# Top-k attention and two MLPs on one core: copies to x, reciprocals and weight stores put later in their queues

## What is computed

```python
scores = q @ k.T / sqrt(64)                       # per head, 576 x 576
kth    = np.partition(scores, -32)[..., -32:-31]   # the 32nd largest of each row
scores = np.where(scores >= kth, scores, -1e9)
attn   = exp(scores - max); attn /= attn.sum(-1) + 1e-9
x      = (attn @ v), heads side by side            # 2304 x 512
gate   = sigmoid(x @ w_gate); val = x @ w_val      # w: 512 x 1536
x      = (gate * val) @ w_out                      # 1536 x 512
h      = x @ w_in                                  # 512 x 2048
out    = relu(h)**2 @ w_out2                       # 2048 x 512
```

## Time and profile before

| | |
|---|---|
| median of 3 runs | 1241.93 us |
| the profiled execution's own time | 1240.17 us |
| its span, first to last instruction | 1238.4 us |
| busy: TensorE / VectorE / ScalarE / GpSimd | 94% / 68% / 60% / 51% of the span |
| mean granted TensorE clock | 0.983 of full speed |

### The profile page before, as it was taken

How to read it: one execution, slowest core, us unless ns; L and a number is a source line. 1 busy time by engine, 2 the same in 40 slices (tenths; PEclk the granted TensorE clock), 3 DMA queues, 4 the chain that set the end, 5 groups by cost and what they waited for, 6 DMA issues and landing times.

```text
span 1238.4 us, 21824 instructions
## 1 busy us (share of the span) xinstructions
PE 1163.2 (94%) x7520; PEld 1004.4 (81%) x7520; DVE 841.3 (68%) x1756; ACT 741.5 (60%) x1758; POOL 628.2 (51%) x539
## 2 busy tenths in 40 slices
PE   3559999989989999999999999999999999999999
PEld 2337888978878999998987777777887888899998
DVE  7788898776678779899967867996565767001140
ACT  5677778766576677677665556765455466112130
POOL 4776678675476456366545434654254256112030
PEclk9969999999989999999999999999999999999999
DMA  9677777776666867665755455556454454577774
GB/s 358 246 259 228 266 258 238 273 270 239 229 245 224 303 201 240 203 218 186 232 192 182 164 190 170 190 184 212 151 199 154 164 170 159 182 241 255 251 256 145
DMA packets 90397, 270.13 MB, mean 218 GB/s; under 512 B 10032, under 2 KB 16176, under 8 KB 90288
## 3 DMA queue, kind: packets, MB, share of 16 engines
q1 hardware_dynamic: 90288, 268.74, 64.5%
HBM read 228.33 MB, written 40.37 MB: 217 GB/s over the span
## 4 chain that ended last, share of the span: by engine, by line
PE 78%; ACT 8%; POOL 5%; issue 3%; DMA 2%; DVE 1%; SPq 1%; ACTq 0%; POOLq 0%
PE ps L582 19%; PE ps L584 18%; PE ps L583 18%; PE ps L523 7%; PE ps L568 7%; PE ps L484 5%; PE ps L500 4%; POOL below L828 2%; DMA wring<-w_in 2%; ACT below L619 2%; ACT scores L614 1%; ACT below L626 1%; POOL ring L823 1%; ACT probs L633 1%; POOL full_buf L868 1%
## 5 line engine op out<-in xcount | busy, mean ns | idle before, releaser
L828 POOL TENSOR_TENSOR below<-scores,below 128x576 f32<-128x576 f32 x144 | 205.5, 1427 | 274.4 <-ACT below L626 273.6
L762 DVE MAX8 top<-work 128x8 f32<-128x576 f32 x432 | 312.2, 750 | 5.0
L582 PE MATMUL ps<-xy_hi,ring 128*128 128x512 f32 (+2 forms) x800 | 290.1, 363 | 4.4 <-ACT act_buf L692 2.4
L584 PE MATMUL ps<-xy_hi,ring 128*128 128x512 f32 (+2 forms) x800 | 282.1, 353 | 0.0
L583 PE MATMUL ps<-xy_lo,ring 128*128 128x512 f32 (+2 forms) x800 | 281.6, 352 | 0.0
L764 DVE MATCH_REPLACE8 work<-top,work 128x576 f32<-128x576 f32 x288 | 213.9, 743 | 0.0
L582 PE MATMUL ps<-g_hi,ring 128*128 128x384 f32 (+2 forms) x560 | 202.8, 362 | 2.7 <-POOL g_lo L857 2.7
L584 PE MATMUL ps<-g_hi,ring 128*128 128x384 f32 (+2 forms) x560 | 198.0, 354 | 0.0
L583 PE MATMUL ps<-g_lo,ring 128*128 128x384 f32 (+2 forms) x560 | 197.7, 353 | 0.0
L833 POOL TENSOR_TENSOR probs<-probs,rinv 128x576 f32<-128x576 f32 x128 | 154.9, 1210 | 62.8 <-DVE rinv L777 62.7
L582 PEld LDWEIGHTS ps<-xy_hi,ring 128*128 128x128 f32 x800 | 150.7, 188 | 24.1 <-issue 6.2
(11 more groups left out here) (58 smaller groups left out, 1723.9 us busy)
## 6 DMA issues: line engine op xcount, KB each, us to landing
ring<-w_split SPq DMA_DIRECT2D x318, 512.0 KB, 3.8
wring<-w_in SPq DMA_DIRECT2D x113, 256.0 KB, 4.2
w_split<-stage SPq DMA_DIRECT2D x46, 512.0 KB, 4.6
w_split<-ring SPq DMA_DIRECT2D x22, 512.0 KB, 3.0
vt<-v_in SPq DMA_DIRECT2D x16, 480.0 KB, 4.6
heads_in<-qk_in SPq DMA_DIRECT2D x16, 336.0 KB, 4.4
vt<-v_in SPq DMA_DIRECT2D x16, 320.0 KB, 3.4
heads_in<-qk_in SPq DMA_DIRECT2D x16, 304.0 KB, 4.2
```

The source lines that it names most:

```text
L582: nc.tensor.matmul(dst, w_hi, hi[:, k, 0:WIDTH[c]], start=first, stop=False)
L584: mm = nc.tensor.matmul(dst, w_lo, hi[:, k, 0:WIDTH[c]], start=False, stop=final)
L762: nc.vector.max(out=best, in_=sc if step == 0 else wk).then_inc(sel_step[t % 2], 1)
L828: nc.gpsimd.tensor_tensor(out=below[:, t % 2, :], in0=scores[:, t % PLACES, :], in1=below[:, t % 2, :], op=ALU.subtract).then_inc(mask_don ...
```

## The change

Three edits, none of which adds or takes away an operation.

- SyncE: the store of a block split on the way goes out at block k for job k + AHEAD - STORE_LAG = k + 2, where it was k + 5.
- ScalarE, slots before 15: `copy_x` of the unit whose product TensorE makes in slot s stood at the end of slot s; it now stands in slot s+1 behind `find_below` and `enlarge`. The last unit of chunk 0 (slot 14) stays.
- VectorE, slots from 15 on: `invert` (the reciprocal) stood behind the first two steps of the selection and ahead of the MLP's work left from the slot before; it now stands behind that work and behind the third step. Slots before 15 had that order already.

```diff
@@ mlp_dma (SyncE) @@
-                    if k + AHEAD in SPLIT_OF and JOBS[k + AHEAD][0] == NW:
-                        store_parts(k + AHEAD)
+                    done = k + AHEAD - STORE_LAG
+                    if done in SPLIT_OF and JOBS[done][0] == NW:
+                        store_parts(done)
@@ ScalarE, slots before MLP_AT[0] @@
                     enlarge(s - MASK)
+
+                if s - 1 in PROD_AT:
+                    copy_x(PROD_AT[s - 1])
                 if s - 1 in SCORE_AT:
                     for t in tiles_of(SCORE_AT[s - 1]):
                         copy_scores(t)
-                if s in PROD_AT and s == MLP_AT[0] - 1:
+                last = s == MLP_AT[0] - 1
+                if last:
                     copy_pt(PROD_AT[s])
                 if 0 <= s - MASK:
                     exp(s - MASK)
-                if s in PROD_AT and s < MLP_AT[0] - 1:
+                if s in PROD_AT and not last:
                     copy_pt(PROD_AT[s])
                 for k in SPLIT_AT.get(s, []):
                     split_weights(k)
-                if s in PROD_AT:
+                if last:
                     copy_x(PROD_AT[s])
@@ VectorE @@
                 select_both(s, [0, 1])
-                if s in NORM_AT and s >= MLP_AT[0]:
-                    invert(NORM_AT[s])
                 for c, n in blocks_of(SHARES[s - 1][2]) if s else []:
                     evac(c, n)
                 select_both(s, [2])
-                if s in NORM_AT and s < MLP_AT[0]:
+                if s in NORM_AT:
                     invert(NORM_AT[s])
```

## The result

| kernel | median us | runs | ratio to the kernel before, 95% interval |
|---|---|---|---|
| before | 1246.32 | 6 (1241.38 to 1248.59) | 1 |
| all three edits | 1237.78 | 6 (1237.31 to 1238.64) | 0.9939 [0.9916, 0.9962] |

The change is faster by 0.4 to 0.8%, 5 to 10 us. The forecast was 1216 us, a gain of 24, with a range of 1206 to 1230: too much, by a factor of three. The profiled execution of the kernel before took 1240.17 us, 6 us under that median; rows of a trace are compared with it in mind.

What follows compares the result with a forecast made beforehand. TensorE was taken as the bound except before 96 us, where ScalarE's loop sets the pace, and in chunk 1's MLP. 1240.2 - 18 (stores) - 8.5 (copies) + 2 (reciprocals) gave 1216 us, range 1206 to 1230.

Steps and rivals of the forecast that it cites:

- What bounds the kernel: TensorE bounds it except before 96 us and in chunk 1's MLP, 240 to 425 us; elsewhere the edits only harm.
- Copies to x: Before slot 15, moving seven copies frees ScalarE's loop of waits: 8.5 us gained, bounds 9.5 and 3.
- Stores: Chunk 1's MLP: later stores let weight loads land in time, cutting TensorE's idle and low clock: 18 us gained, 5 to 23.
- the loads were hidden anyway: Rival: TensorE's chunk 1 stops have other reasons close behind, so stores give 5 us, 1229 in all; chance 0.17.
- Its sign: Sign of a wrong forecast: chunk 1 still stops behind ScalarE although no load is late; no size given.
- The warning: In chunk 1, ScalarE waited for late loads 11 times, TensorE for its copies only 8: not tied one to one.
- the store's own cover: SyncE's ring: the store has three blocks, 8 us, before its place is loaded again, and takes 2.9 us: covered.
- Reciprocals: From slot 15, later normalisations make four of 72 turns short, 3.3 us: 2 us lost, bounds 1 gained to 8 lost.
- The two rules of the Trainium skill: Loaded HBM access slows chunk 1's weight loads, 5 us less; VectorE and GpSimd exclude each other in SBUF, 2 us more.
- The sum: Whole kernel: 1240.2 - 18 - 8.5 + 2 = 1215.7, so 1216 us.
- the two gains: Stores in chunk 1, 18 us, and copies to x before 96 us, 8.5 us.
- the base: The whole kernel's profiled execution, 1240.2 us, taken as starting time, 1.8 us under the median of 1241.93.

Runs made afterwards that it cites:

- the fastest: ScalarE's copies of the turned unit ahead of left MLP work, against copies and stores moved, early reciprocals, GpSimd's normalisation behind its left MLP work: 1214.58 us, 0.9746.
- the slowest: Only the reciprocals moved later, from slot 15 on, against the kernel before: 1258.47 us, 1.0092.

## Why the prediction was wrong

- **What bounds the kernel**: right. Time was to be had ahead of 96 us and in chunk 1, and elsewhere the edits could only harm. They did harm: 5.7 us idle for 2.2 between 425 and 625 us. (One reading is off: no row gives the 165 us behind the shares of 84% and 74%. Of TensorE's busy 168 us they are 82% and 72%, which changes nothing.)
- **Copies to x**: right in mechanism and size, 8.5 us foreseen, 10 measured [8, 12], the stage 7.4 us shorter in the pair of traces and 8.4 in the mean of all.
- **Stores**: the mechanism was right (every wait named fell as foreseen), the term was too large, 18 us for 14 [12, 16]. The step that failed was taking all idle time over that of the neighbouring stretches for the loads' fault. Only 5 of the 16.6 us were; for the other 11.5 the mechanism of the rival "the loads were hidden anyway" was right, though its price of 5 us in all was not. Its sign came true too: chunk 1 still stops behind ScalarE although hardly a load is late, 8.2 us of waits for the turned unit with all edits where the earlier trace rows had 9.7. The warning, 11 late loads for 8 waits of TensorE, was in the rows and should have weighed more. Moving GpSimd's normalisation found 4 us of the rest; for the last 7 no run gives the reason. On the store's own cover the text says once "6 blocks behind block k" and once three: at block k the store is that of k + 2, and its place is loaded again at block k + 3, three blocks on. It landed in 5.5 us there and not in 2.9, SyncE waited 25.8 us for landings, and by the run with the store at k + 3 such waits had no price that can be told.
- **Reciprocals**: the step that failed most: "I take 2 us lost", with 8 as the bound; measured 11 alone [9, 13] and 13 beside the others. The turns cost 3.4 us as worked out. But the sum priced only the one waiter that the data names. The earlier trace rows shows GpSimd idle for 1.95 us before its normalisation, and in GpSimd's list the squares, the low parts and the weight splits of the MLP and the next tile's subtraction stand behind it. Where GpSimd already stood waiting, the delay was added to its queue, 78 us in all, and from there it reached ScalarE and TensorE. Its own bound of 8 us was too low for the same reason. And the granted clock was lower where TensorE stopped more: 5.9 us more of busy time for the same matmuls beside the other edits, 4.1 alone.
- **The two rules of the Trainium skill.** By the one ("DMA: Bandwidth & Descriptors", "Latency and other measured facts") ScalarE would have kept waiting in part for the weights. The loads did land later, between 232 and 418 us in 4.4 us with all edits and 5.3 with the stores alone, where it was 3.7. But with the store at k + 3 it was 3.8, and with it at k + 2 in the otherwise same kernel 5.8, both at a DMA share of 0.79, so the share alone doesn't set it. Of ScalarE's 18.7 us of waits 2.5 are left, 4.5 with the stores alone, so the rule was worth little here. By the other ("SBUF — State Buffer", "Who interferes with whom") the late normalisation would have been lengthened beside VectorE's subtractions, for 2 us. The trace shows nothing of it: the 128 normalisations of the earlier trace rows took 154.9 us in all before and 154.3 with all edits.
- **The sum**: 1246 - 10 - 14 + 11 gives 1233, by the three edits measured alone; together they gave 1238, as the reciprocal costs 13 and copies and stores 21 for 24 in company. Of the 22 us between the forecast and 1238, 11 are the reciprocals (13 for 2), 5.5 the two gains (21 for 26.5), and 6 the base: 1240.2 was the time of one execution, and the median of six was 1246. With the reciprocals at 11 the forecast would have read 1225, with the stores at 14 as well 1229. The range was too narrow by its own terms, too: its upper end took 12, 5 and 4 us for them, while the bounds that the text gives, 5, 3 and 8, make it 1240.2 - 5 - 3 + 8 = 1240.

## What to carry to other kernels

When an instruction is moved later in an engine's list, its price isn't the slack of the one that needs its result. Look at the engine that waits for it: is it already idle in front of that wait, and what stands behind it in its queue, and who waits for those? When a late event and a stall occur in the same stretch, count the pairs before giving the whole stall to it. And where a wait for data must stay in a shared queue, put work that is ready ahead of it: here this single move gave 8 us, not much less than each of the three edits moved the time by.

## What the hardware showed that I had not expected

Beside the waits, the granted clock moves time. Behind the first MLP matmul TensorE does the same matmuls in every kernel here, and was busy for 1110.6 us in the fastest and 1121.6 us in the slowest. Less idle time mostly goes with a higher clock, but the total doesn't settle it. Between 232 and 418 us the kernel with stores only idles 11.5 us at 0.99, that with copies and stores as much at 0.97, all three edits 13.8 us at 0.94, and the reciprocals alone 24.1 us at 0.95. These are single profiled executions, and no run here pins down what does settle it.
